# New routing without sorted buffers, w1 copied by ScalarE, and a block-diagonal second copy of the attention's state

## The reference

```python
for t in range(S):
    y[:, :, t] = np.einsum('bhd,bhde->bhe', rt, state)
    Sa = np.einsum('bhde,bhe->bhd', state, at)
    state_decay = state * wt[:, :, None, :] - np.einsum('bhd,bhe->bhde', Sa, bt)
    state = state_decay + np.einsum('bhd,bhe->bhde', vt, kt)
...
x = np.ascontiguousarray(y.transpose(0, 2, 1, 3)).reshape(B * S, H * D)
# layer 1 of 2: expert = argmax of x @ w_gate; out = softmax weight * sigmoid(x @ w_output_gate)[expert]
#               * (relu(x @ w1[e]) @ w2[e])
# layer 2 of 2: the same without the output gate, and each expert takes at most 768 tokens, in token order
```

## Time and profile before

| what | value |
|---|---|
| median of 3 runs | 1363.74 us |
| time of the profiled execution | 1370.99 us |
| its span, first to last instruction | 1369.1 us |
| mean granted clock of TensorE | 0.85 |
| busy: PE, PEld, DVE, ACT, POOL | 79%, 67%, 34%, 19%, 26% |
| chain that ended last | PE 74%, issue 9%, POOL 5%, DVE 5%, DMA 4%, ACT 2% |

### The profile page before, as it was taken

The page is one execution under the profiler, slowest core; times in us unless marked ns, Lnnn a source line. Parts: engine busy times, 40 slices in busy tenths (PEclk is TensorE's granted clock), DMA queues, the critical chain, the costliest instruction groups (busy, mean ns, idle before and its releaser), DMA issues.

```text
span 1369.1 us, 45453 instructions
## 1 busy us (share of the span) xinstructions
PE 1079.5 (79%) x19760; PEld 915.0 (67%) x19761; DVE 471.5 (34%) x891; ACT 262.4 (19%) x524; POOL 353.6 (26%) x302
## 2 busy tenths in 40 slices
PE   1287777887887888850999999997713999998996
PEld 1277777777787777620888888885303888886884
DVE  7554434534455332250223233231140232322321
ACT  0143333433333333210111011110100110100100
POOL 4443043313444210007112212121034122111211
PEclk8577787787877877885899999999856999999998
DMA  2344543435444221223133333332412313344110
GB/s 80 90 104 114 119 115 93 128 108 122 111 100 125 66 44 48 79 81 116 30 107 109 105 110 109 107 115 61 136 46 85 103 40 110 113 125 157 33 29 1
DMA packets 158724, 125.79 MB, mean 92 GB/s; under 512 B 91498, under 2 KB 136046, under 8 KB 158576
## 3 DMA queue, kind: packets, MB, share of 16 engines
q1 hardware_dynamic: 139216, 93.56, 25.0%
q10 hardware_dynamic: 12096, 14.09, 3.5%
q0 software_dynamic: 7264, 15.86, 3.4%
HBM read 89.60 MB, written 36.16 MB: 92 GB/s over the span
## 4 chain that ended last, share of the span: by engine, by line
PE 74%; issue 9%; POOL 5%; DVE 5%; DMA 4%; ACT 2%; SPq 1%; POOLq 0%; ACTq 0%; DVEq 0%
PE pair L1175 18%; PE pair L1156 16%; PE pair L1163 5%; POOL x_sorted L606 4%; PE bank L1026 3%; PE bank L939 2%; PE pair L1118 2%; PE pair L845 2%; PE pair L1143 2%; PE pair L862 2%; PE bank L1034 2%; PE pair L908 2%; PE pair L879 2%; PE pair L1008 2%; PE pair L894 2%
## 5 line engine op out<-in xcount | busy, mean ns | idle before, releaser
L1175 PE MATMUL pair<-abk_in,H_nat 128*128 x992 | 279.1, 434 | 1.8 <-DVE y_T L1439 1.7
L1156 PEld LDWEIGHTS pair<-y_T,rvm 128*128 128x128 f32 x1984 | 238.1, 197 | 19.7 <-issue 7.2
L1156 PE MATMUL pair<-y_T,rvm 128*128 128x128 f32 x1984 | 239.4, 281 | 8.6 <-DVE rvm L1424 6.3
L1175 PEld LDWEIGHTS pair<-abk_in,H_nat 128*128 128x128 f32 x992 | 183.7, 190 | 72.9 <-issue 3.0
L792 ACT ACTIVATE H_nat<-pair 128x512 f32<-128x512 f32 x62 | 37.0, 597 | 527.0 <-PE pair L1163 527.0
L1424 DVE COPY rvm<-AG 128x2560 f32 x62 | 97.1, 1567 | 96.4 <-issue 74.6
L1143 PE MATMUL pair<-table_sb,y_T 128*128 128x128 f32 x186 | 34.6, 296 | 92.9 <-DMA y_T<-x_sorted 92.9
L554 POOL TENSOR_TENSOR AG<-abk_in,F_run 40x512 f32<-40x512 f32 x48 | 60.4, 1259 | 175.5 <-DVE T_nat L1257 156.1
L568 POOL TENSOR_SCALAR_AFFINE_SELECT AG<-AG 64x512 f32<-64x512 f32 x48 | 54.9, 1145 | 179.7 <-ACT AG L647 177.3
L1431 DVE TENSOR_SCALAR H_nat<-pair 128x512 f32<-128x512 f32 x62 | 42.7, 688 | 147.8 <-PE pair L1163 147.8
L606 POOL DMA_INDIRECT x_sorted<-x_all,slot_i x48 | 50.5, 1053 | 146.8 <-DVE x_all L1415 132.8
(11 more groups left out here) (140 smaller groups left out, 1498.8 us busy)
## 6 DMA issues: line engine op xcount, KB each, us to landing
abk_in<-w SPq DMA_DIRECT2D x16, 1280.0 KB, 8.5
y_T<-x_sorted ACTq DMA_DIRECT2D x62, 160.0 KB, 2.3
AG<-w SPq DMA_DIRECT2D x16, 512.0 KB, 3.6
AG<-w SPq DMA_DIRECT2D x32, 256.0 KB, 4.5
x_sorted<-empty SPq DMA_DIRECT2D x6, 1288.0 KB, 8.1
t_dram<-T_rows SPq DMA_DIRECT2D x12, 384.0 KB, 2.5
AG<-w SPq DMA_DIRECT2D x32, 128.0 KB, 5.0
w_in<-wT SPq DMA_DIRECT2D x48, 80.0 KB
```

The source lines that it names most:

```text
L1156: mm(to, w1_now[:, par, k * F + m * P:k * F + m * P + P], xT[:, (0, 2 - m // 4)[k], :], start=(m % 4 == 0 and k == 0), stop=False, skip_gr ...
L1175: last = mm(bank[5][:, 0:DM], hidT[par][:, k, :], ring2[:, bass.ds(place, 1), k, :].rearrange("p a d -> p (a d)"), start=(k == 0), stop=(k ...
```

## The change

- **State twice.** `state_out` writes the new state also into `Z_diag`, with the two heads of a pair as diagonal blocks of one 128 x 128 square. `state_natural` is then 8 products with 104 moving columns in place of 16 with 40; `state` opens with 2 products of 320 columns in place of 16 of 40; `outputs` has 8 products with `S_nat` in place of 16. `s_out` is one copy of 128 x 832 in place of two of 40 x 320.
- **Logits of layer 0 in the attention.** `turn_y` multiplies by a matrix `turns` that carries the router's columns beside the identity (8 fp32 products of 104 columns in place of 8 transposes). `x_out` has a third copy, of the logit parts, which VectorE sums (`lg_sum`). The tokens are written to DRAM (`x_dram`) from ScalarE's queue, two DMAs a set.
- **No sorted buffers.** The clearings go. The routing computes for each slot its token and gate with 24 products of one-hot matrices (`in_place`, `carried`), and POOL gathers each tile's rows by indirect DMA, three tiles ahead, in both layers. POOL's load of gate and token number per tile goes.
- **Logits of layer 1 in layer 0.** VectorE multiplies each result tile by the second router's weights (broadcast to all partitions, 128 x 2,560 elements) and reduces; the logits are stored beside the rows and loaded together, 3,072 runs of 32 bytes. The second router is turned once in DRAM, in pieces of 4 bytes.
- **Counts.** One scan of 192 replaces eight of 24; six products of 512 columns whose result is not used (`WARM`) stand behind the count's.
- w1's copy moves from VectorE to ScalarE, behind the rectifying and the copy of x. The expert loops are unrolled. The ring of w1 has memory of its own, and expert 0's load no longer waits for the last copy of x. Result rows have two buffers.

```diff
             def s_out(u):
                 act.wait_ge(sn_ready, u + 1)
-                for o in range(2):
-                    copy(S_nat[head_rows(o), u % 2, o].rearrange("p b a d -> p (b a d)"),
-                         pair[0][head_rows(o), o, 0:H * D], sn_copied)
+                copy(S_nat[:, u % 2, :, :, 0:SPAN],
+                     pair[0][:, :, :].rearrange("p b (a x) -> p b a x", x=P)[:, :, :, 0:SPAN], sn_copied)
...
@@ state_natural
+                if state_source(u) >= 0:
+                    pe.wait_ge(z_kept, 2 * states_upto(state_source(u)))
...
                     for a in range(NPAIR):
-                        at = (b * NPAIR + a) * D
-                        for o in range(2):
-                            q, rows = head_rows(o), half_rows(o)
-                            last = mm(pair[0][q, o, at:at + D], ZV[rows, u % 4, o, b, a, :], eyes[rows],
-                                      start=True, stop=True)
+                        last = mm(pair[0][:, b, a * P:a * P + SPAN], Z_diag[:, diag_of(u), b * NPAIR + a, :],
+                                  ident[:, 0:SPAN], start=True, stop=True)
...
@@ state
-                        for o in range(2):
-                            mm(bank[7][head_rows(o), at:at + D], S_nat[:, u % 2, o, b, a, :], eyes,
-                               start=(a == 0 and b == 0), stop=False, skip_group_check=True)
+                for o in range(2):
+                    mm(bank[7][head_rows(o), 0:H * D], ident[:, SIDE[o]:SIDE[o] + D],
+                       Z_diag[:, diag_of(u), :, SIDE[o]:SIDE[o] + D], start=True, stop=False, skip_group_check=True)
...
@@ outputs
-                        for o in range(2):
-                            mm(bank[6][head_rows(o), at:at + C], S_nat[:, u % 2, o, b, a, :],
+                        mm(bank[6][0:SPAN, at:at + C], S_nat[:, u % 2, b, a, 0:SPAN],
...
@@ turn_y
-                        last = nc.tensor.transpose(pair[2][:, b, a * P:(a + 1) * P], y_T[:, b, a, :], ident)
+                        last = mm(pair[2][:, b, a * P:a * P + SPAN], y_T[:, b, a, :], turns[:, a, :],
+                                  start=True, stop=True)
...
@@ VectorE, state_out
+                dve.wait_ge(z_cleared, 1)
+                for o in range(2):
+                    q = head_rows(o)
+                    v.tensor_tensor(
+                        Z_diag[q, diag_of(to), :, SIDE[o]:SIDE[o] + D], view(7, 2 * NPAIR, D)[q],
+                        end_decay[q, k, c::CC].unsqueeze(2).to_broadcast([D, 2 * NPAIR, D]), ALU.mult
+                        ).then_inc(z_kept, 1)
...
@@ POOL, per layer
+                def gather(i):
+
+                    if i >= AHEAD:
+                        pool.wait_ge(L["xt_ready"][s], i - AHEAD + 1)
                     pool.indirect_dma_start(
-                        out=x_sorted[s],
-                        out_offset=bass.IndirectOffsetOnAxis(ap=slot_i[:, t:t + 1], axis=0),
-                        in_=x_all[:, t, :], in_offset=None).then_inc(L["scattered"][s], 16)
...
+                        out=x_rows[i % AHEAD][:, 0:(DM, ROW)[s]], out_offset=None, in_=source_of[s],
+                        in_offset=bass.IndirectOffsetOnAxis(ap=token_all[:, s, i:i + 1], axis=0),
+                        bounds_check=last_token, oob_is_err=False).then_inc(x_landed[s][i % AHEAD], 16)
...
+                if s == 1:
+                    for n in range(2):
+                        pool.wait_ge(o_stored[0][n], 16 * tiles_by(MT, n))
+                    pool.dma_start(lg_all[:, :, 0:E], between[:, DM:ROW].rearrange("(t p) e -> p t e", p=P)
+                                   ).then_inc(lg_landed, 16)
...
@@ ScalarE, per tile
+                    if i + 1 < MT:
+                        relu0(i + 1, (i + 1) % 2)
+                    if i + 2 < MT:
+                        x_turned(i + 2)
+                    if i + 3 < MT:
+                        stage_w1(i + 3, (i + 3) % 2)
...
@@ TensorE, routing
+                for g in range(NG):
+                    if g % (NG // PARTS) == 0:
+                        pe.wait_ge(L["place_set"][s], g // (NG // PARTS) + 1)
+                    last = mm(bank[6][:, 0:2 * MT], in_place[:, g, :],
+                              carried[:, g, :, :].rearrange("p n m -> p (n m)"),
+                              start=(g == 0), stop=(g == NG - 1))
...
@@ VectorE, per tile of layer 0
+                def next_logits(i):
+                    dve.wait_ge(L["o_copied"][s], i + 1)
+                    if i:
+                        dve.wait_ge(lg_made, i)
+                    v.tensor_tensor(terms, wr_next[:, :, :],
+                                    y_rows[i % 2][:, 0:DM].unsqueeze(1).to_broadcast([P, E, DM]), ALU.mult
+                                    ).then_inc(terms_made, 1)
+                    dve.wait_ge(terms_made, i + 1)
+                    v.tensor_reduce(y_rows[i % 2][:, DM:ROW], terms, AX_X, ALU.add).then_inc(lg_made, 1)
```

More of the change, by code:

```diff
@@ L99, in tables @@
     t["eyes"][64 + d, d] = 1
+    for at in range(NPAIR):
+        t["turns"][d, at * SPAN + d] = 1
+        t["turns"][64 + d, at * SPAN + 64 + d] = 1
     j, i = np.arange(P)[:, None], np.arange(P)[None, :]
@@ L233, in recurrence_and_experts @@
+        upto, rank = (part(G_flat, n * NG * E, E, NG) for n in (3, 4))
+        above = part(G_flat, 5 * NG * E, E, N // P)
+        past = part(G_flat, 6 * NG * E, MT, E - 1)
+        in_place = part(F_flat, 0, NG, P)
+        in_tile = part(F_flat, NG * P, NG, MT)
+        carried = part(T_flat, 0, NG, 2, MT)
+        x_rows = [y_flat[:, n * ROW:(n + 1) * ROW] for n in range(AHEAD)]
+        y_rows = [S_flat[:, n * ROW:(n + 1) * ROW] for n in range(2)]
         hidT = [part(H_flat, n * F, FC, P) for n in range(2)]
-        empty = sb("empty", [P, ROW])
@@ L625, in send @@
[L625 to L639 removed]
+                        out_offset=bass.IndirectOffsetOnAxis(ap=token_all[:, s, i:i + 1], axis=0),
@@ L642, in _ @@
+                        in_=y_rows[i % 2][:, 0:(ROW, DM)[s]], in_offset=None, bounds_check=last_token,
+                        oob_is_err=False).then_inc(o_stored[s][i % 2], 16)
+                for i in range(AHEAD):
+                    gather(i)
+                for i in range(MT):
+                    if i + AHEAD < MT:
+                        gather(i + AHEAD)
+                    send(i)
         @block.scalar
```

472 lines of the change are left out of this document (216 added, 256 removed).

## The result

Four runs of the changed kernel gave 1272.08 us by median (1261.69 to 1287.04), four of the kernel before beside them 1364.12. The ratio is 0.9299 (95% interval 0.9241 to 0.9357): 7% faster. The forecast was 1237, its range 1175 to 1285. The time lies in the range, but 35 us above the forecast and next to the rival "own work" (1268). The profiled execution took 1287.04 us (span 1285.3), is the longest of the four and counts as a slow one, so the ratio leaves it out; in which stage its 15 us above the median lie is not known.

The account below looks back on a forecast made before the run. TensorE's products were taken to bound the experts, and products plus waits for the instruction stream the attention. Attention -23, first routing -56.3, between layers -51.4, experts +4.2 sum to -126.5: 1363.74 becomes 1237 us, range 1175 to 1285.

Parts of the forecast that it names:

- own work: Attention: stream no bound, or second state's writes waited for; attention +8, up to +25; 1268, up to 1285; chance 0.20.
- Sign and size: Whole kernel: faster by more than 0.2% (2.7 us), chance 0.96; forecast 1237 us.
- Attention, products: Attention: 112 of 1,288 matmul records a set fewer, some of them wider; -10 us, ends -40 and +21.
- between two limits, the middle: Attention products: -40 if the instruction stream sets the pace, +21 if TensorE's work does; -10 taken.
- Attention, turning of the router: Attention: one-off turning in 4-byte pieces, 3 to 30 us on the queues, TensorE feeling a part: +3.
- Attention, clearings: Attention: eight clearings of the sorted tokens go, 2 us each: -16 us (0 to -26).
- Attention, sum: Attention: products -10, clearings -16, router's turning +3: -23 us (-65 to +25).
- First routing: Attention's last transposes to first expert product: 26.2 us in place of 82.5, -56.3 (-50 to -61).
- Between the layers: Layer 0's last product to layer 1's first: 47.7 us in place of 99.1, -51.4 (-25 to -58).
- Experts: Layer 0: VectorE's logits hidden, tile still 9.45 us; layer 1: w1 copies on ScalarE delay products, +4.2 us.
- The clock rises: Attention: wider products and fewer waits raise TensorE's clock; -82 us there, 1178 in all; chance 0.18.
- VectorE never became the bound: Rival, layer 0's experts: VectorE's logits stretch a tile from 9.45 to 14.1 us; +144, 1381; chance 0.04.

Follow-up runs that it names:

- the base: Changed kernel with the router's turning after the attention's last slot and 10 warm products in place of 6: 1270.62 us, ratio 0.9279.
- the old state: The base with natural copy, opening and reading of the state as before the change: 1263.55 us, ratio 0.9211.

## Why the prediction was right or wrong

**Sign and size.** The forecast faster by more than 0.2% held, and the time lies in the range, but the mechanism of its largest uncertain term did not hold. By medians the sum missed by 35 us; between the two profiles it missed by 43, of which the attention's term is 44.

**Attention, products: wrong.** The step that failed is the price of a record "in proportion to its moving columns": 0.091 us for 104, 0.056 for 64. In the base the natural copy's 16 records take 2.03 us at the high clock and 3.74 at the low one, where I had 1.45 and 2.9; the reading's 16 take 1.60 and 2.91, 0.100 each at the high clock and not 0.056; the turned outputs' 16 take 2.03 in place of 1.45. The natural copy's and the outputs' records, at 0.127, cost somewhat more than a record of the experts' first group (0.112), and what all of these have in common is 104 to 128 columns of weights. The removed narrow products were cheap: 31 records of the old natural copy in 0.77 us are 0.025 each, below even the 0.035 that 40 moving columns cost by my price. In the code two of them use different rows and columns of the array; that they run side by side for this reason is an inference. By the section "LDWEIGHTS (loading the stationary operand)" of the Trainium skill's page "TensorE: Matmul & The Clock Gate" a weight load takes its columns over 1.2, in ns, whatever its rows: 107 ns for 128 columns, 87 for 104. The trace has the same order: 0.112 and 0.127 us a record for 128 columns, and 0.100 for the reading's 104. That the weights set these times follows from the rows and was not tested by itself. My "between two limits, the middle" then failed in the same direction: the stream gave less (18 of 310 us, by estimate 27 in the whole attention, where I had 40 as its most) and own work more (27 of 310 us, by estimate 40, against 28, and in my 28 the turned outputs are counted too). The second state leaves +7 us, seen twice on taking it out. My -10 also held the turned outputs, which no run takes out: 2.03 us a group in place of 1.09 at the high clock is some 11 us of TensorE's time in 12 sets, where I had 5.

**Attention, turning of the router: mis-sized.** Taken at +3 of "3 to 30". Moving it to the end gains 16; the attention itself is held up by some 20, and by 21 to 24 when it is split. I had reasoned that TensorE would feel "a part" of the queues' time; it feels nearly all, through two ways that I had not followed: its own instruction packets, and the landing of the solve's rows.

**Attention, clearings: right within its bounds.** -11 in place of -16.

**Attention, sum.** The three terms that experiments measured are +7 + 16 - 11 = +12, against -23; the two profiles show +21. Between them stand, as far as is known, the 4 to 6 us by which the turning's 20 exceed what moving it gains, and the turned outputs. With the turning behind the attention and the old state, the last record of the turned outputs starts at 567.1 us, before the change at 569.5, although some 11 us of clearings are gone: by estimate 9 us of other cost remain. These are single profiles of different occasions, good to some 6 us.

**First routing: right but for a missing term.** -50.4 against -56.3. VectorE's chain was right to 0.2 us, and gather and turning took 5.5 us, 6.3 forecast. The 6.5 us behind them are the placing products at the low clock, which stood in no term.

**Between the layers: right by luck, through two errors.** 47.0 us against 47.7. The logits' load was 5 us cheaper than priced, and the placing products, 6.5 us, stood in no term.

**Experts: right in mechanism and in size, hidden by another gain.** The period is still 9.45 us, and VectorE is hidden (two passes at 2.82 us where I had 3.05). ScalarE's copies of w1, 2.34 us, do delay TensorE in layer 1, as the waits in the base show and as their removal by VectorE's copies confirms (4 to 6 us). TensorE's waits in layer 1, before and after:

```profile
PE pair L1156 <- DVE rvm L1424: 6.3, 2, 3.3
...
PE pair L1160 <- ACT H_nat L665: 10.7, 4, 4.8
```

From its first product to the end of its last, layer 1 went from 307.5 to 310.9 us: +3.4, where I had +4.2. What stands behind the last product went from 12.1 to 8.0 us, which my sum did not have: 1.6 us of it is the way to the last scatter, before which VectorE had to wait for POOL's load of gate and token number, now gone; the rest was not followed up. So the stretch came out 0.9 us shorter and not 4.2 longer.

**Sum.** The stretches of the two profiles add up to -84, the medians of the runs give 1272.1 - 1364.1 = -92. The 8 us between them are the 15 by which the profiled execution after lies above its median, less the 7 by which the one before does. In which stages they arise is not shown, so a closer agreement of terms and medians would be chance.

**Rivals.** "Own work" (1268, chance 0.20) is what happened in the time and nearly in the cause, and its +8 for the attention was nearer than my -23. But it had 21 for the products, of which the second state's measured part is 7, and 3 for the turning, of which 16 was measured, and its reason, that the stream is no bound, is not what the waits show ("issue" fell from 82 to 63 us). "The clock rises" is half true: it is 0.79 with the old state and 0.85 with the second one, and the attention still gains nothing, since TensorE is also busy longer, 220 us of 250 in place of 208. VectorE never became the bound.

## What to carry to other kernels

Count a product's price by both of its operands: a few products with wide weights can cost more than twice their number of narrow ones on different parts of the array (16 records in 2.03 us against 31 in 0.77), even where the instruction stream is a visible bound. Give a DMA of thousands of 4-byte pieces its full time wherever other engines fetch instructions or wait for small transfers, and look for a slot in which nobody waits; cutting it into eight showed no gain here, and loading it in contiguous pieces was not tried. Products whose only work is to keep the clock up must reach until the data are ready: ending 3.6 us early took all of their effect, and 1 us early most of it (10.50 and 8.79 us against 5.5).

## What the runs showed of the hardware

- 2,560 pieces of 4 bytes from DRAM to DRAM take some 26 to 31 us from issue to the load that waits for them (556.5 to 582.6, 577.3 to 605.8, 570.9 to 601.5), and let one instruction packet through in 25 us. A transfer on another queue landed after 21.4 us in place of 2.4.
- Splitting such a DMA into eight, one in each of eight slots, showed no gain: the sets were 3 us longer each (45.3 against 41.9 and 42.3), 21 to 24 in seven sets, against 20 for the one piece.
- The same 48 records took 5.47 to 5.57 us where TensorE had stood idle at most 0.6 us before them, 8.79 at a granted clock of 0.61 behind 0.96 us, and 10.50 at 0.50 behind 3.6 us.
- A denser stretch was granted a higher clock (0.85 against 0.79, TensorE busy 220 and 208 of 250 us) with fewer instructions in it, and was not faster.
- The same two kernels stood at a ratio of 0.930 on one occasion and of 0.940 on another, each with an interval of 0.004 to 0.006 to either side.
